# An attention stage in another order on all engines, with 64x64 grams and loads issued earlier

## The reference

```python
# 1: delta-rule attention, batch 2, 8 heads, 768 tokens, head size 48
k_n = k / (norm(k) + 1e-6)
for t in range(768):
    y[t]  = q[t] @ state
    state = state + beta[t] * outer(k_n[t], v[t] - state.T @ k_n[t])
# 2: on the 1536 rows of y (width 384): h = x @ w_in (384 x 1024)
sm = softmax(h); solu = h * sm
ln = (solu - mean(solu)) / sqrt(var(solu) + 1e-6) * g_ln
x  = ln @ w_out                       # 1024 x 384
# 3: top-1 mixture of 8 experts, capacity 384:
#    out[i] = gate * relu(x[i] @ w1[e]) @ w2[e]
```

## Time and profile before

| | us |
|---|---|
| median of 3 runs | 473.42 (473.24 to 477.04) |
| the profiled execution | 475.6 |
| its span, first to last instruction | 473.9 |
| attention(0) starts / mlp(0) starts | 61.30 / 98.68 |
| attention(1) starts / mlp(1) starts | 144.93 / 172.97 |
| attention(2) starts / mlp(2) starts | 219.00 / 246.16 |
| layer 3 starts | about 286.65 |

### The profile page before, as it was taken

How to read it: one execution, slowest core, us unless ns; L and a number is a source line. 1 busy time by engine, 2 the same in 40 slices (tenths; PEclk the granted TensorE clock), 3 DMA queues, 4 the chain that set the end, 5 groups by cost and what they waited for, 6 DMA issues and landing times. The chain is left out here.

```text
span 473.9 us, 13934 instructions
## 1 busy us (share of the span) xinstructions
PE 401.1 (85%) x5935; PEld 379.3 (80%) x5936; DVE 302.5 (64%) x559; ACT 218.3 (46%) x389; POOL 80.0 (17%) x81
## 2 busy tenths in 40 slices
PE   2357589699999979999979991589999998999992
PEld 2356588588999868999868990589999998999991
DVE  4799558749946678972523727676956956455650
ACT  1333621137762114772113742356866865456650
POOL 3400200000060000050000002431332332301102
PEclk9999999769999989999989997579999999899997
DMA  6795100339510059010032017817357557161000
GB/s 136 264 203 177 32 3 4 71 67 233 185 36 19 5 127 200 26 36 21 4 79 57 0 52 267 308 47 284 140 189 284 161 194 284 45 257 44 19 7 24
DMA packets 27879, 54.39 MB, mean 115 GB/s; under 512 B 4468, under 2 KB 21424, under 8 KB 27344
## 3 DMA queue, kind: packets, MB, share of 16 engines
q1 hardware_dynamic: 23648, 48.04, 33.5%
q0 software_dynamic: 3136, 4.73, 3.2%
q10 hardware_dynamic: 1040, 0.79, 0.8%
HBM read 44.30 MB, written 9.44 MB: 113 GB/s over the span
## 5 line engine op out<-in xcount | busy, mean ns | idle before, releaser
L1357 PE MATMUL PS<-xTh,w1h 128*128 128x256 f32 (+1 forms) x192 | 57.8, 301 | 3.5 <-DVE xTl L1265 1.8
L1359 PE MATMUL PS<-xTh,w1l 128*128 128x256 f32 (+1 forms) x192 | 57.2, 298 | 0.0
L1358 PE MATMUL PS<-xTl,w1h 128*128 128x256 f32 (+1 forms) x192 | 57.2, 298 | 0.0
L968 PE MATMUL PS<-w_in_h,mlpT 128*128 128x512 f32 x144 | 50.4, 426 | 3.3 <-DMA mlpT<-yT 3.3
L1357 PE MATMUL PS<-w2h,hTh 128*128 128x384 f32 x136 | 46.1, 339 | 0.0
L1359 PE MATMUL PS<-w2h,hTl 128*128 128x384 f32 x136 | 45.5, 335 | 0.0
L1358 PE MATMUL PS<-w2l,hTh 128*128 128x384 f32 x136 | 45.5, 335 | 0.0
L1271 DVE SCALAR_TENSOR_TENSOR hTl<-PS,hTh 128x384 fp32r<-128x384 f32 x64 | 35.3, 552 | 10.4 <-ACT hTh L1131 9.9
L1357 PEld LDWEIGHTS PS<-xTh,w1h 128*128 128x128 f32 x192 | 38.3, 199 | 4.5 <-issue 2.1
L1300 POOL DMA_INDIRECT out<-yo,oiu x24 | 23.9, 997 | 105.0 <-ACT yo L1142 79.7
L1131 ACT ACTIVATE hTh<-PS 128x384 fp32r<-128x384 f32 x64 | 31.7, 495 | 17.7 <-PE PS L1359 17.3
(11 more groups left out here) (174 smaller groups left out, 892.5 us busy)
## 6 DMA issues: line engine op xcount, KB each, us to landing
w1r<-w SPq DMA_DIRECT2D x8, 1536.0 KB, 6.4
w2r<-w SPq DMA_DIRECT2D x8, 1536.0 KB, 10.4
KP<-kv SPq DMA_DIRECT2D x3, 1536.0 KB, 11.8
mlpT<-yT SPq DMA_DIRECT2D x12, 288.0 KB, 4.0
QT<-qt SPq DMA_DIRECT2D x6, 384.0 KB, 6.3
out<-zero SPq DMA_DIRECT2D x12, 192.0 KB, 3.9
x<-rowst SPq DMA_DIRECT2D x12, 192.0 KB, 1.9
yT<-w_out_t SPq DMA_DIRECT2D x1, 1536.0 KB, 6.5
```

What stands on the lines that cost most here:

```text
L968: last = pe.matmul(PS[:, h_bank(n) + s, :], mlpT[:, n, x, c, :], w[:, c, o], start=(c == 0 and j == 0), stop=(c == KD - 1 and j == 2))
L1357: pe.matmul(out_ap, lhs[0], rhs[0], start=first, stop=False)
L1358: pe.matmul(out_ap, lhs[0], rhs[1], start=False, stop=False)
L1359: return pe.matmul(out_ap, lhs[1], rhs[0], start=False, stop=final)
```

## The change

All engines' lists of attention are rewritten; what is computed stays the same.

- `grams`: one 64x64 product per chunk and head in place of 32x64 and 32x32. The diagonal block of the odd 32-block then stands in columns 32 to 63, so it is copied to columns 0 to 31 in PSUM before `systems` transposes: `odd_blocks` on ACT (for group 0 one block on ACT and one on DVE).
- `gram_blocks` is split in `roots` and `cross_blocks`. In attention(0) ACT does odd_blocks(2) before state(2) and cross_blocks(2) after it; roots(2) moves into mlp(0).
- The masking of the scores moves from POOL to DVE: for group 0 `mask_first` multiplies `PT` in place, for the others `mask_scores` reads the scores from PSUM in two halves and ACT's `take_scores` is gone from there.
- PE: solve in the order 1, 0, 3, gate(0), 2; both outputs of the first half before advance(1); grams(2) after output_inner(2); output_state(2) and output_inner(3) before advance(3). In mlp, `scores` one place later.
- DVE: `lower(g+1)` before solution(1); `fold_steps` one, two and three places among the queries; `step_matrix` split in `query` and `step_matrix`; in attention(0) `w_in_low` before state(0); `state(3)` in mlp. `w_out_l` (the split of w_out) after lower_block(0).
- Loads: SP waits for `kk` >= 4 (of now four signals, all grams of group 0 as before); `w_out_t` lies in `XE`, so the load of w_in waits no more; the copy `w_in_h` on ACT moves behind solution(0, 0).

```diff
-                sp.wait_ge(kk, 8)
+                sp.wait_ge(kk, 4)
...
                 load_kv(0)
-                sp.wait_ge(wfold, 1)
                 sp.dma_start(w_in_raw, ...).then_inc(ld_const, 16)
...   # scalar
+                def odd_blocks(g):
+                    act.wait_ge(kk, 4 * (g + 1))
+                    for c in range(1 if g == 0 else 2):
+                        b = block(2 * c + 1)
+                        last = act.activation(grams_at(g)[b, :, 0:BL], grams_at(g)[b, :, BL:CH], ACT.Copy)
+                    last.then_inc(a_od, 1)
...
                 def attention(g):
+                    later = g + 2 < GROUPS
                     solution(g, 0)
+                    if g == 0:
+                        w_in_high()
                     solution(g, 2)
                     state(g, 0)
-                    state(g, 1)
                     y_high(g, 0)
                     y_high(g, 1)
+                    state(g, 1)
+                    move_x(g, 0, row_pieces()[PIECES // 2:PIECES])
+                    if later:
+                        odd_blocks(g + 2)
                     state(g, 2)
-                    move_x(g, 0, row_pieces()[PIECES // 2:PIECES])
+                    if later:
+                        cross_blocks(g + 2)
+                    y_high(g, 2)
                     state(g, 3)
-                    if g + 2 < GROUPS:
-                        gram_blocks(g + 2)
-                    y_high(g, 2)
                     y_high(g, 3)
...   # vector
                 def systems(g):
-                    dve.wait_ge(kk, 8 * (g + 1))
+                    dve.wait_ge(kk, 4 * (g + 1))
+                    if g == 0:
+                        link(dve.tensor_copy(grams_at(0)[block(3), :, 0:BL], grams_at(0)[block(3), :, BL:CH]))
+                    dve.wait_ge(a_od, g + 1)
                     dve.transpose(As[:], ...)
...
+                def mask_first():
+                    dve.wait_ge(e_pt, 1)
+                    dve.tensor_tensor(PT, PT, later_c[:, :].unsqueeze(1).to_broadcast([P, NU, CH]), ALU.mult).then_inc(masked, 2)
+
+                def mask_scores(g, par):
+                    dve.wait_ge(qk, 4 * (g + 1))
+                    dve.wait_ge(uy, 2 * NC * g)
+                    dve.tensor_tensor(PT[:, HP * par:HP * par + HP], scores_at(g, par), later_c[:, :].unsqueeze(1).to_broadcast([P, HP, CH]), ALU.mult).then_inc(masked, 1)
...   # tensor
-                        for q in range(P // BL):
+                        for c in range(2):
                             for par in range(2):
-                                o = chunk(q // 2) if q % 2 == 0 else block(q)
-                                w = CH if q % 2 == 0 else BL
-                                last = pe.matmul(grams_at(g)[block(q), HP * par + i, 0:w], ...)
+                                tokens = KT[g % 2][half(par), i, chunk(c)]
+                                last = pe.matmul(grams_at(g)[chunk(c), HP * par + i], tokens, tokens, start=True, stop=True)
...   # tensor, attention(g), from gate(g, 1) on
                     gate(g, 1)
+                    output(g, 0)
+                    output(g, 1)
                     advance(g, 1)
-                    output(g, 0)
                     inflow(g, 1, 0)
                     inflow(g, 1, 1)
-                    output(g, 1)
                     advance(g, 2)
                     output_inner(g, 2)
-                    advance(g, 3)
                     if g + 2 < GROUPS:
                         grams(g + 2)
                     output_state(g, 2)
-                    output(g, 3)
+                    output_inner(g, 3)
+                    advance(g, 3)
+                    output_state(g, 3)
```

More of the change, by code:

```diff
@@ L331, in strictly_lower @@
                     pool.affine_select(out=Ts, in_=As[:], compare_op=ALU.is_gt, fill=0.0, base=0, pattern=[[1, BL], [-1, BL]], channel_multiplier=0).then_inc(below, 1)
[L333 to L338, removed]
                 strictly_lower(0)
-                later_only(0)
                 pool.wait_ge(consts2, 4)
+                pool.wait_ge(below, 1)
                 clear_t(0)
@@ L345, in _ @@
                 for g in range(1, GROUPS):
-                    later_only(g)
+                    pool.wait_ge(below, g + 1)
                     clear_t(g)
@@ L514, in fold, with w_in_high @@
                     act.activation(w_out_h[:], w_raw, ACT.Copy).then_inc(w_hi, 1)
+                def w_in_high():
                     act.wait_ge(ld_const, 16)
@@ L637, in attention @@
                         scales(g + 1)
+                        lower(g + 1)
                     solution(g, 1)
                     if ahead:
[L640 removed]
+                        fold_steps(3)
+                    solution(g, 3)
+                    query(g, 0, 0)
                     step_matrix(g, 0, 0)
+                    query(g, 0, 1)
                     step_matrix(g, 0, 1)
[L643 to L644 removed]
                     if g == 0:
                         w_in_low()
[L647 to L648 removed]
+                    if ahead:
+                        fold_steps(2)
+                    query(g, 1, 0)
+                    state(g, 0)
+                    step_matrix(g, 1, 0)
+                    query(g, 1, 1)
+                    if ahead:
+                        fold_steps(1)
+                    y_low(g, 0)
                     state(g, 1)
[L650 removed]
+                    y_low(g, 1)
                     step_matrix(g, 1, 1)
[L652 removed]
                     if ahead:
[L654 to L662 removed]
                         rows_of_t(1)
                         rows_of_t(2)
+                    state(g, 2)
                     if g + 2 < GROUPS:
                         systems(g + 2)
+                    if ahead:
+                        rows_of_t(3)
                     y_low(g, 2)
@@ L691, in _ @@
                 dve.memset(St[:], 0.0).then_inc(s_clear, 1)
-                dve.wait_ge(const_ready, 4)
+                dve.wait_ge(const_ready, 5)
                 for par in range(2):
-                    last = dve.tensor_copy(eye2[half(par)], ident[half(par), half(par)])
+                    dve.tensor_copy(eye2[half(par)], ident[half(par), half(par)])
+                last = dve.tensor_copy(later_c[chunk(1)], later[chunk(1), chunk(1)])
                 last.then_inc(s_clear, 1)
@@ L720, in _ @@
                     if ahead:
-                        rows_of_t(3)
+                        rows_of_t(4)
                     mlp_max(g, 0)
                     if ahead:
-                        rows_of_t(4)
+                        rows_of_t(5)
                     mlp_mul(g, 0)
                     mlp_max(g, 1)
-                    if ahead:
-                        rows_of_t(5)
+                    state(g, 3)
                     mlp_max(g, 2)
```

98 lines of the change are left out of this document (48 added, 50 removed).

## The result

The changed kernel takes **456.03 us** (median of 4 runs, 452.13 to 458.91) against 475.23 (473.24 to 477.29, 4 runs) for the kernel before in the same comparison: a ratio of 0.959 (95% interval 0.950 to 0.968), some 19 us faster. As a gain over the kernel before, which is the fairer measure since that kernel's median moved from 473.42 to 475.23, 11.3 us were forecast and 19 measured.

The account below looks back on a forecast made before the run. PE bounds the mlp; front and attention are chains through several engines, with PE instruction refills. -9.2 up to the gate, -2.6 attention(0), +0.5 attention(1), 0 elsewhere: -11.3 from 473.4 gives 462, range 456.5 to 470.

Parts of the forecast that it names:

- the stalls that go with half as many instructions: Front, grams(0): half the instructions avoid the 4.10 us stall, ending at 9.2 instead of 13.35, -4.2 us.
- the inversion that POOL slowed: Front, DVE's inversion: without POOL's mask, operations of 768 and 512 elements take 1.0 and 0.7 us, -3.6 us.
- the price of `w_out_l`: Before gate(0): its 3.38 us on DVE behind lower_block give back 1.1 us of the gain.
- Its one stall: Front, `between`: one refill of PE's instruction stream, 0.6 us of stall (0 to 4).
- a gap of over 2 us between fold and solve: Front, PE: new "issue" gaps of over 2 us there would show the forecast wrong.
- the new wait: Attention(0): PE's output_state(2) waits for ACT's copy of state(2), behind two copies, 2.6 us.
- PE waits for it 1.9 us: Attention(1): PE waits for the copy of state(2) behind rows_of_t(1) and (2); the stage changes by +0.5 us.
- terms put at nothing: Attention(2) 0 (-1 to +1) and mlp 0 (0 to +1); layer 3 not touched.
- Rival A: Attention(0) and front: refill fits, PE stays at 2.4 GHz, grams run at 16.4 ns; about 457, chance 0.13.
- B: Half gained: attention(0) gives back +2 and +2, attention(1) and (2) lose 1.5 each; 469, chance 0.15.
- C: Front: four refills after fold each stall 4.1 us beside earlier loads; 478, slower, chance 0.06.
- D: Front does not move since fold waits for w_out; attention(0)'s 2.6 less 0.5 stays; 471, chance 0.06.

Follow-up runs that it names:

- after: The changed kernel with the whole change, against the kernel before: 456.03 us, ratio 0.959.
- b: The changed kernel with the old 32x64 and 32x32 grams and no copies of odd blocks; ratio to the kernel before 0.9835.
- c: The changed kernel with the mask of group 0's scores back on POOL; ratio to the kernel before 0.9629.
- d: The changed kernel with w_out_l moved to before DVE's copy of lower_block(0) for solve; ratio to the kernel before 0.9532.
- after_again: The changed kernel, unaltered, run once more in a later set; 455.03 us, ratio to the kernel before 0.9568.
- a: The changed kernel with output_state(2) also waiting for the state after chunk 2; 462.53 us, ratio to the kernel before 0.9705.
- i: The changed kernel with w_out_l ahead of lower_block(0) and a separate semaphore for fold's loads; 454.96 us, ratio to the kernel before 0.9525.
- j: The kernel before with the 64x64 grams and their copies, w_out_t in XE and no wait for wfold; 463.44 us, ratio 0.9745.
- k: The changed kernel with the old order of attention on PE, DVE and ACT; 463.21 us, ratio to the kernel before 0.9724.
- f: The kernel before with the loads alone: w_out_t in XE and no wait for wfold; ratio 0.9998.
- h: The changed kernel with a separate semaphore for w_out_t and w_gate, so fold need not wait for w_out; 455.78 us, ratio to the kernel before 0.9452.
- g: The changed kernel with PE's old order alone in the middle of attention, DVE's and ACT's left new; ratio to the kernel before 0.9956.

## Why the prediction was off

The steps, against the first profile of after:

| step | forecast | measured |
|---|---|---|
| DVE's first transpose | 10.6 | 10.54 |
| 768-element operation | 1.0 | 0.96 |
| fold starts | 24.9 | 24.67 |
| stall in `between` | 0.6 | 1.80 |
| solve | 51.0 | 51.64 |
| gate(0) | 57.9 | 58.53 |
| first move of rows | 73.6 | 72.90 |
| refill in grams(2) and behind | 1.5 | 1.37 |
| PE's wait for the state after chunk 2 | 2.6 | 0 |
| mlp(0) | 86.9 | 83.82 |
| attention(1) | +0.5 | -0.4 |
| attention(2), mlp | 0 | -0.7, -1.6 in three |
| layer 3 | 0 | -1.7 (varies in unchanged code) |

**Right** were the front with both its causes: the stalls that go with half as many instructions (b), the inversion that POOL slowed (c), and the price of `w_out_l` (d). The sum up to the gate is 0.6 us off. Its one stall was set too short: 1.80, and 2.53 in after_again's profile, where 0.6 was charged and a gap of over 2 us between fold and solve was named as a sign that the whole was wrong; that sign is met there and the reading of the refills stands all the same. Two slips in the working behind the gate are small and opposed: 16.5 + 0.9 - 1.5 is 15.9 and not 15.7, and three outputs of 1.1 with an advance of 0.9 are 4.2 and not 4.3.

**The step that failed** is "Then comes the new wait: state(2) on ACT is behind two copies that wait for these grams: 2.0, with its own copy and the semaphores 2.6", and with it "PE waits for it 1.9 us" in attention(1). The copy is as late as forecast (it starts at 80.28 in after), but output_state(2) does not read it. The chart of who is late was right and that of who is waiting was wrong; the number in the wait line, one less than assumed, decides. Run a puts the wait in and gets the forecast's waits and its start of mlp(0). The wait is worth about 5.5 to 6.5 us between after (0.957 to 0.959) and a (0.9705), more than the 4.5 us that the two waits were charged, as the slow matmuls behind it come on top. It is most of the 8 us that the forecast lacks, but not all. The rest are terms put at nothing: attention(2) and mlp, -0.7 and -1.6 in after's first profile, and layer 3.

**Rival A** was the nearest, at 457 with a chance of 0.13, but mostly by luck. One of its three parts holds: PE enters mlp(0) at full speed. The refill in and behind grams(2) did not vanish, as the 1.5 us of its first part wanted, but took 1.37, about what the forecast had; and grams(0) ran at 28.8 ns. What spoke against A was the wait that doesn't exist, and most of what brought the time near 457 is that wait's price. **B** falls: nothing was given back behind the gate. **C**, refills of 4 us beside the earlier loads, shows only where the old grams stay: 4.49 and 5.20 in b. With the new ones the worst before solve is 1.80 in after, 2.53 in after_again and 2.73 in i. **D** falls, with fold at 24.67.

**The parts.** Grams alone bring 7 us, the loads alone 0, both 12, and the order 7.5 more. Grams and loads together gain 5 us that neither brings alone. What the masks on DVE gain and `w_out_l` gives back lies, with the changes in mlp, between j (0.9745) and k (0.9724): 1 us, which the runs do not tell from nothing.

**What stays open** is why a refill varies from run to run. The one in `between` took 1.80 in the first profile of after, 2.53 in the second and 1.26 in a, with the same instructions ahead of it. These 1.3 us are a part only of the runs' spread, 452 to 459. Open too is which piece of the new order shortens attention(2) and mlp(2), in a as in after.

## What to carry to other kernels

When a producer moves back in a list, read the consumer's wait as a number before pricing it: which copy of the buffer does it ask for? An output needs the state that enters its chunk, not the one that leaves it. Count instructions as well as columns: many tiny matmuls run no faster than the instruction stream comes in, and larger tiles can win with the array no faster at all. Price a wait with the slow matmuls behind it: 2 us of idle cost more than 2 us here. Where two limits hide each other, the part tried alone may show nothing, so try the pair before it is dropped.

## What the runs showed of the chip

PE's stalls without a visible cause stand at fixed places of the program. In the earlier trace rows the last two lie 256 instructions apart, and between the first two the trace has 766, about three times as many. With 768 instructions fewer in all (three times 128 matmuls and as many weight loads), 512 of them ahead of `between`, the stall there is where it was: `between` breaks after 45 and before 83 matmuls in both kernels. The traffic of the instruction queue fell with it, from 46 packets in the page of before; of after:

```profile
q8 instruction: 43, 0.70, 0.7%
```

Three packets fewer for 768 instructions are one for every 256. The pages of all runs agree: 46 packets with the old grams (before, b and f), 43 with the new in every other. 0.70 MB in 43 packets are 16 KB each. The Trainium skill (Runtime: NRT & Kernel Launch, Instruction fetch mechanics) has such blocks but calls a crossing mostly hidden. The runs agree only where PE waits for something else: at c's 6.07 and h's 8.29 us for `T1u` no stall is seen in `between`, while b loses 4.49 and 5.20 in the middle of fast matmuls.

The second thing is how much a short idle costs PE once it runs at full speed. After 2.57 us of waiting in a the granted clock is 0.50 over the 6.57 us of outputs behind it, and still 0.50 in the first 2.3 us of mlp(0). After 2.46 in k and 2.13 in g it fell as well; in after, where PE lost 1.02 and 1.02 us in the same part of attention(0), it stayed at 1.00.
